# Moving the rounded activations of an fp32 matmul chain by 64 bytes within 256, with every other tensor kept at its byte

## Chip, cores and metric

One core of one Trainium2 chip runs the whole program in one launch. The metric is device time in microseconds (us), median over runs, and lower is better. Before the change it is 638.91 us, the median of 3 runs that lie between 638.78 and 639.15.

## What is computed

Three stages follow each other: windowed attention, a mixture of 4 experts with shares, and a block with a cosine. All data are fp32.

```python
# attention: 2 batches, 8 heads, 576 tokens, head size 64, each token sees itself and 63 before it
attn = softmax(where(mask, q @ k.T / 8, -1e9)); x = (attn @ v)        # as 1152 tokens x 512
p = domain_probs / (domain_probs.sum(-1) + 1e-9)                      # 1152 x 4
out = sum over e of p[:, e] * (relu(x @ w1[e]) @ w2[e])               # w1: 512 x 1024, w2: 1024 x 512
h = out @ w_in                                                        # w_in: 512 x 2048
result = (h * cos(h)) @ w_out                                         # w_out: 2048 x 512
```

## The kernel before

**Split products.** A weight or an activation `a` is held as two tensors of type float32r, a rounded part `a_hi` and what is left, `a_lo = a - a_hi`. A product `a b` is then three matmuls into one PSUM bank: `a_hi b_hi`, `a_hi b_lo` and `a_lo b_hi`. ScalarE writes the `_hi` tensors with a copy, VectorE or GpSimd writes the `_lo` tensors with a subtraction.

**The tensors.** `w_hi` and `w_lo` hold the 8 chunks (of 128 hidden units) of one block of weights, in 1024 columns each: 512 for the way up and 512 for the way down. `x_hi` and `x_lo` hold the tokens: 4 slices of 128 channels, 1152 tokens each. `hp_hi` and `hp_lo` hold the hidden values of four chunks for 384 tokens. For three of the experts, pairs of chunks are multiplied by a scheme with 7 products for 8 (`pair_product`). It needs sums of token blocks, `t_hi` and `t_lo`, and sums of weight blocks, `ex_hi` and `ex_lo`.

**The matmuls.** All of them have a stationary operand of 128 columns, which a weight load brings into the array, and a moving operand which is streamed through it.

- Up (`up_cells`, line 1270): stationary is a 128-column piece of `w`, moving are 384 tokens of `x`. A hidden chunk takes 12 matmuls (4 slices by 3).
- Up in pairs (`pair_product`, line 1314): stationary is a piece of `w` or `ex`, moving are 384 tokens of `x` or `t`. A product takes 6 matmuls.
- Down (`down_cells`, line 1297, and `pair_outputs`, line 1328): here the roles are the other way round. Stationary are 128 tokens of `hp`, moving are the 512 down columns of `w`. A hidden chunk takes 9 matmuls.

In a matmul the trace names the moving operand first: `bank<-x_hi,w_hi` is moving `x_hi` by stationary `w_hi`. Once the attention is done, TensorE goes to and fro between two chunks up (24 matmuls) and two chunks down (18), the down ones LAG = 3 chunks behind, so that ScalarE and VectorE have time to turn a bank into `hp_hi` and `hp_lo`. The order is written out by hand. Each engine has its own list of instructions, and semaphores join them.

**Where tensors lie.** SBUF tensors follow each other in the order in which they are declared, each start rounded up to 32 bytes. The first one, `w_hi`, starts at byte 16512 of each partition, that is at byte 128 modulo 256. `w_hi`, `w_lo`, `w_raw`, `x_hi` and `x_lo` are whole multiples of 256 bytes long, and so are all pieces into which matmuls cut them (512-byte pieces of `w` and `hp`, 1536-byte pieces of `x` and `t`). So each operand starts at the byte of its tensor, modulo 256.

Of the kernel before, what the change touches and what calls it, by code (L numbers as in the profile page):

```python
# [27 lines left out]
P = 128  # L28
# [12 lines left out]
E = 4  # L41
# [7 lines left out]
TILES = N // P  # L49
# [60 lines left out]
def build(nc, q, k, v, probs, weights, out):  # L110
    with ExitStack() as ctx:
        def sb(name, shape, dt=F32):
            return ctx.enter_context(nc.sbuf_tensor(name, shape, dt))
# [4 lines left out]
        w_hi = sb("w_hi", [P, FC, 2 * DM], F32R)  # L118
        w_lo = sb("w_lo", [P, FC, 2 * DM], F32R)
        w_raw = sb("w_raw", [P, STAGE, 2 * DM])  # L120
        x_hi = sb("x_hi", [P, DC, N], F32R)
        x_lo = sb("x_lo", [P, DC, N], F32R)
        p_tok = sb("p_tok", [P, E, TILES])
        half_pi = sb("half_pi", [P, 1])
        hp_hi = sb("hp_hi", [P, HP, TOK], F32R)
        hp_lo = sb("hp_lo", [P, HP, TOK], F32R)
        h_raw = sb("h_raw", [P, HP, TOK])
        p_now = sb("p_now", [P, NTOK, OC])
        ident = sb("ident", [P, P])
        mask = sb("mask", [P, 3, P])  # L130
        zeros = sb("zeros", [P, P])
# [25 lines left out]
        with ExitStack() as sums:  # L157
            def sum_sb(name, *shape):
                t = sums.enter_context(nc.sbuf_tensor(name, [P, *shape], F32R))
                return t[(slice(None),) * (len(shape) + 1)]  # L160

            t_hi = sum_sb("t_hi", 3, 2, TOK)
            t_lo = sum_sb("t_lo", 3, 2, TOK)
            ex_hi = sum_sb("ex_hi", GROUPS, EX * P)
            ex_lo = sum_sb("ex_lo", GROUPS, EX * P)
        c_u, c_k, c_r1, c_r2, c_abs, c_cos = (
# [1423 lines left out]
```

## Time and profile before

| | |
|---|---|
| median of 3 runs | 638.91 us |
| the profiled execution | 638.61 us, of which the span of instructions is 636.6 us |
| TensorE matmuls | 99% of the span, 3658 instructions |
| TensorE weight loads | 88% |
| VectorE, ScalarE, GpSimd | 47%, 41%, 43% |
| DMA | 36.73 MB in its main queue, 18.1% of the 16 engines' time |

Matmuls are pipelined, so one's duration in the trace (some 335 or 390 ns) is longer than the time from its start to the start of the next. That time, called the step below, is what a matmul costs in a stream, and it is read from starts in the timeline, or from the length of a run of matmuls in the chain of waits divided by their number.

### The profile page before, as it was taken

What the parts mean: (1) busy time and instruction counts of PE and PEld (TensorE: products, weight loads), DVE (VectorE), ACT (ScalarE), POOL (GpSimd) and SP (SyncE); (2) the same over time, 40 slices, a digit from 0 to 9 for tenths busy, and PEclk for the clock granted to TensorE, in tenths of its full rate; (3) what the DMA queues carried; (4) which work ended last, traced back from release to release, by engine and by line L of the source; (5) the groups of instructions that cost most, each with busy time, mean ns of one, the idle gap of its engine ahead of it and who ended that gap; (6) DMA issues with size and microseconds to landing.
All of it is one profiled execution on the core that took longest, in us unless ns stands there. A gap on an engine that the chain in (4) does not pass through costs nothing.

```text
span 636.6 us, 10169 instructions
## 1 busy us (share of the span) xinstructions
PE 629.4 (99%) x3658; PEld 562.4 (88%) x3658; DVE 301.9 (47%) x726; ACT 261.0 (41%) x558; POOL 271.7 (43%) x405
## 2 busy tenths in 40 slices
PE   7999999999999999999999999999999999999997
PEld 6877899989899999999998888988999999999996
DVE  5654431215433314432414443426775666766564
ACT  6885312233321223321223321246655467544542
POOL 6892246697710396720396720287000069400000
PEclk9999999999999999999999999999999999999999
DMA  9975000021220021120022220133100012001011
GB/s 271 280 237 187 8 1 0 1 66 67 68 66 1 1 66 66 66 66 0 1 67 66 67 66 1 32 101 100 34 0 1 2 39 94 1 0 49 0 51 50
DMA packets 23432, 37.25 MB, mean 59 GB/s; under 512 B 2784, under 2 KB 16096, under 8 KB 23392
## 3 DMA queue, kind: packets, MB, share of 16 engines
q1 hardware_dynamic: 23392, 36.73, 18.1%
q8 instruction: 24, 0.39, 0.3%
q14 instruction: 16, 0.13, 0.1%
HBM read 34.36 MB, written 2.36 MB: 58 GB/s over the span
## 4 chain that ended last, share of the span: by engine, by line
PE 97%; DVE 1%; DMA 1%; issue 0%; SPq 0%; POOL 0%; ACT 0%; DVEq 0%
PE bank L1270 31%; PE bank L1297 31%; PE bank L1328 16%; PE bank L1314 14%; PE bank L1248 2%; PE bank L1212 1%; PE bank L1237 1%; PE bank L1411 1%; DMA k_t<-in_k 1%; DVE s_sb L878 0%; DVE acc L1058 0%; DVE prob_t L927 0%; PE bank L1221 0%; SPq L322 0%; POOL prob L481 0%
## 5 line engine op out<-in xcount | busy, mean ns | idle before, releaser
L456 POOL TENSOR_TENSOR w_lo<-w_raw,w_hi 128x128 fp32r<-128x128 f32 (+1 forms) x244 | 144.9, 630 | 213.9 <-ACT w_hi L658 212.4
L1270 PE MATMUL bank<-x_hi,w_hi 128*128 128x384 f32 (+1 forms) x384 | 131.3, 342 | 0.0
L1270 PE MATMUL bank<-x_hi,w_lo 128*128 128x384 f32 (+1 forms) x384 | 129.2, 336 | 0.0
L1270 PE MATMUL bank<-x_lo,w_hi 128*128 128x384 f32 (+1 forms) x384 | 128.8, 335 | 0.0
L1297 PE MATMUL bank<-w_hi,hp_hi 128*128 128x512 f32 x288 | 114.8, 399 | 0.1
L1297 PE MATMUL bank<-w_hi,hp_lo 128*128 128x512 f32 x288 | 113.5, 394 | 0.0
L1297 PE MATMUL bank<-w_lo,hp_hi 128*128 128x512 f32 x288 | 112.2, 390 | 0.0
L1011 DVE TENSOR_TENSOR h_raw<-bank,h_raw 128x384 f32<-128x384 f32 x84 | 46.7, 556 | 91.8 <-PE bank L1314 91.7
L1270 PEld LDWEIGHTS bank<-x_hi,w_hi 128*128 128x128 f32 x384 | 72.2, 188 | 2.9 <-issue 0.5
L1270 PEld LDWEIGHTS bank<-x_lo,w_hi 128*128 128x128 f32 x384 | 72.2, 188 | 1.6
L942 DVE SCALAR_TENSOR_TENSOR hp_lo<-bank,hp_hi 128x384 fp32r<-128x384 f32 x48 | 26.5, 556 | 98.5 <-ACT hp_hi L690 57.5
L1270 PEld LDWEIGHTS bank<-x_hi,w_lo 128*128 128x128 f32 x384 | 72.1, 188 | 0.0
L1297 PEld LDWEIGHTS bank<-w_lo,hp_hi 128*128 128x128 f32 x288 | 54.1, 188 | 12.1
L682 ACT ACTIVATE hp_hi<-h_raw 128x384 fp32r<-128x384 f32 x48 | 25.2, 525 | 94.9 <-DVE h_raw L1011 94.9
L1297 PEld LDWEIGHTS bank<-w_hi,hp_hi 128*128 128x128 f32 x288 | 54.1, 188 | 10.8 <-issue 0.4
L1297 PEld LDWEIGHTS bank<-w_hi,hp_lo 128*128 128x128 f32 x288 | 54.3, 189 | 8.5
L1328 PE MATMUL bank<-w_hi,hp_lo 128*128 128x512 f32 x144 | 56.6, 393 | 0.0
L1328 PE MATMUL bank<-w_hi,hp_hi 128*128 128x512 f32 x144 | 56.6, 393 | 0.0
L1328 PE MATMUL bank<-w_lo,hp_hi 128*128 128x512 f32 x144 | 56.2, 390 | 0.0
L658 ACT ACTIVATE w_hi<-w_raw 128x1024 fp32r<-128x1024 f32 x40 | 42.0, 1051 | 11.7 <-PE bank L1297 11.7
L1077 DVE TENSOR_TENSOR h_raw<-c_cos,bank 128x384 f32<-128x384 f32 x48 | 26.6, 554 | 37.0 <-ACT c_cos L753 37.0
L751 ACT ACTIVATE c_abs<-c_r 128x384 f32<-128x384 f32 x48 | 25.2, 525 | 42.6 <-DVE c_r L1069 42.5
(112 smaller groups left out, 970.9 us busy)
## 6 DMA issues: line engine op xcount, KB each, us to landing
w_raw<-in_weights SPq DMA_DIRECT2D x43, 512.0 KB, 3.6
q_t<-in_q SPq DMA_DIRECT2D x12, 192.0 KB, 5.3
result<-acc SPq DMA_DIRECT2D x9, 256.0 KB, 2.1
w_raw<-in_weights SPq DMA_DIRECT2D x8, 256.0 KB, 6.0
k_t<-in_k SPq DMA_DIRECT2D x8, 224.0 KB, 5.6
v_w<-in_v SPq DMA_DIRECT2D x4, 384.0 KB, 4.8
v_w<-in_v SPq DMA_DIRECT2D x4, 320.0 KB, 6.2
k_t<-in_k SPq DMA_DIRECT2D x4, 192.0 KB, 4.4
```

The costliest lines, as they stand in the source:

```text
L456: last = nc.gpsimd.tensor_tensor(w_lo[:, f, at:at + part], raw[:, at - begin:at - begin + part], w_hi[:, f, at:at + part], ALU.subtract)
L658: nc.scalar.activation(w_hi[:, f, :], w_raw[:, f % STAGE, :], ACT.Copy).then_inc(w_hi_done, 1)
L682: nc.scalar.activation(hp_hi[:, i, :], h_raw[:, i, :], ACT.Relu).then_inc(pair_hi_done, 1)
L751: nc.scalar.activation(c_abs, c_r2, ACT.Abs).then_inc(cos_abs, 1)
L942: nc.vector.scalar_tensor_tensor(out=hp_lo[:, f % HP, :], in0=ps[:, 0:TOK], scalar=0.0, in1=hp_hi[:, f % HP, :], op0=ALU.max, op1=ALU.subt ...
L1011: nc.vector.tensor_tensor(h_raw[:, place, :], ps, h_raw[:, other, :], ALU.add).then_inc(pair_taken, 1)
L1077: nc.vector.tensor_tensor(h_raw[:, f % HP, :], c_cos, bank_h, ALU.mult).then_inc(cos_taken, 1)
L1248: last = nc.tensor.matmul(out_cell, v_w[:, r, WINDOW_OF[t][block_of], heads], prob_t[:, h, block_of // 2, at:at + WIN], start=True, stop=True)
L1270: last = nc.tensor.matmul(ps[:, 0:TOK], w[:, f, chunk(c)], x[:, c, token_cols(t)], start=c == 0 and i == 0, stop=c == DC - 1 and i == 2)
L1297: last = nc.tensor.matmul(y_ps[c][:, :], h[:, f % HP, chunk(c)], w[:, f, DM:2 * DM], start=f == 0 and i == 0, stop=f == FC - 1 and i == 2)
L1314: last = nc.tensor.matmul(bank[(g * PRODUCTS + j) % 2][:, 0:TOK], a, b, start=c == 0 and i == 0, stop=c == 1 and i == 2)
L1328: last = nc.tensor.matmul(pair_y[t][c][:, :], h[:, i, chunk(c)], w[:, f, DM:2 * DM], start=f == 0 and k == 0, stop=f == FC - 1 and k == 2)
```

## The change

Empty tensors are declared between others, and two small arrays (`p_tok`, the shares, and `half_pi`, a constant) go from between the tokens and the hidden values to behind `p_now`. No instruction is added, removed or moved on any engine, and shapes, semaphores and DMAs are the same. Only addresses differ.

```diff
         w_raw = sb("w_raw", [P, STAGE, 2 * DM])
+
+        sb("before_x", [P, 16])
         x_hi = sb("x_hi", [P, DC, N], F32R)
         x_lo = sb("x_lo", [P, DC, N], F32R)
-        p_tok = sb("p_tok", [P, E, TILES])
-        half_pi = sb("half_pi", [P, 1])
+        sb("before_hp", [P, 32])
         hp_hi = sb("hp_hi", [P, HP, TOK], F32R)
         hp_lo = sb("hp_lo", [P, HP, TOK], F32R)
         h_raw = sb("h_raw", [P, HP, TOK])
         p_now = sb("p_now", [P, NTOK, OC])
+        p_tok = sb("p_tok", [P, E, TILES])
+        half_pi = sb("half_pi", [P, 1])
+        sb("before_ident", [P, 16])
         ident = sb("ident", [P, P])
@@
+            sum_sb("before_t", 16)
             t_hi = sum_sb("t_hi", 3, 2, TOK)
             t_lo = sum_sb("t_lo", 3, 2, TOK)
+            sum_sb("before_ex", 48)
             ex_hi = sum_sb("ex_hi", GROUPS, EX * P)
             ex_lo = sum_sb("ex_lo", GROUPS, EX * P)
```

The starts that follow, in bytes of a partition modulo 256 (modulo 512 in brackets):

| tensors | before | after |
|---|---|---|
| `w_hi`, `w_lo`, `w_raw` | 128 (128) | 128 (128) |
| `x_hi`, `x_lo` | 128 (128) | 192 (192) |
| `t_hi`, `t_lo` | 128 (384) | 192 (192) |
| `ex_hi`, `ex_lo` | 128 (384) | 128 (384) |
| `hp_hi`, `hp_lo`, `h_raw`, `p_now` | 64 (320) | 64 (320) |
| `ident`, `mask`, `zeros`, `acc`, `q_t`, `k_t`, `v_w`, `s_sb`, `prob`, `prob_t`, `c_u` to `c_cos` | 128 (384) | 128 (128) |
| `p_tok` | 128 (128) | 128 (384) |

Moving less stationary, modulo 256, is therefore 0 before and 64 after in the up matmuls and in the pair products, and 64 both before and after in the down matmuls (`w` at 128 by `hp` at 64).

## Rows read from the trace of the kernel before

**Rows 1.** The page: span, TensorE's busy time, and its granted clock in 40 slices
```profile
span 636.6 us, 10169 instructions
...
PE 629.4 (99%) x3658; PEld 562.4 (88%) x3658; DVE 301.9 (47%) x726; ACT 261.0 (41%) x558; POOL 271.7 (43%) x405
...
PEclk9999999999999999999999999999999999999999
```
**Rows 2.** The page's chain that ended last, by engine and line
```profile
PE 97%; DVE 1%; DMA 1%; issue 0%; SPq 0%; POOL 0%; ACT 0%; DVEq 0%
PE bank L1270 31%; PE bank L1297 31%; PE bank L1328 16%; PE bank L1314 14%; PE bank L1248 2%; PE bank L1212 1%; PE bank L1237 1%; PE bank L1411 1%; DMA k_t<-in_k 1%; DVE s_sb L878 0%; DVE acc L1058 0%; DVE prob_t L927 0%; PE bank L1221 0%; SPq L322 0%; POOL prob L481 0%
```
**Rows 3.** Waits of TensorE: us in total, times, longest us
```profile
PE bank L1453 <- DVE zeros L858: 1.2, 1, 1.2
PE bank L1221 <- POOL prob L481: 0.7, 1, 0.7
PE bank L1212 <- DMA k_t<-in_k: 0.7, 1, 0.7
...
```
**Rows 4.** Groups of TensorE's instructions: count, busy us and mean ns, idle us
```profile
L1270 PE MATMUL bank<-x_hi,w_hi 128*128 128x384 f32 (+1 forms) x384 | 131.3, 342 | 0.0
...
L1297 PE MATMUL bank<-w_hi,hp_hi 128*128 128x512 f32 x288 | 114.8, 399 | 0.1
...
L1314 PE MATMUL bank<-x_hi,ex_hi 128*128 128x384 f32 x48 | 16.2, 337 | 0.0
L1314 PE MATMUL bank<-x_hi,w_hi 128*128 128x384 f32 x48 | 16.2, 337 | 0.0
...
L1314 PE MATMUL bank<-t_hi,w_hi 128*128 128x384 f32 x24 | 8.3, 345 | 0.0
```
**Rows 5.** The chain in order of time: start us, length us, line, matmuls in it
```profile
264.84 4.21 PE bank L1314 x24
...
391.80 4.17 PE bank L1270 x24
...
502.65 4.12 PE bank L1297 x18
506.77 4.19 PE bank L1270 x24
510.96 4.12 PE bank L1297 x18
```
**Rows 6.** Timeline of TensorE, one run up and one down: start us, length us
```profile
506.61 0.33 PE L1270 MATMUL bank<-x_hi,w_hi 128*128 128x384 f32 x1
506.78 0.34 PE L1270 MATMUL bank<-x_lo,w_hi 128*128 128x384 f32 x1
...
507.68 0.33 PE L1270 MATMUL bank<-x_hi,w_hi 128*128 128x384 f32 x1
...
510.80 0.39 PE L1297 MATMUL bank<-w_hi,hp_hi 128*128 128x512 f32 x1
...
514.92 0.33 PE L1270 MATMUL bank<-x_hi,w_hi 128*128 128x384 f32 x1
```
**Rows 7.** Timeline of the weight loads beside the first two of them
```profile
506.62 0.19 PEld L1270 LDWEIGHTS bank<-x_lo,w_hi 128*128 128x128 f32 x1
506.79 0.19 PEld L1270 LDWEIGHTS bank<-x_hi,w_lo 128*128 128x128 f32 x1
```
**Rows 8.** Groups of other engines that read or write the moved tensors
```profile
L530 POOL TENSOR_TENSOR h_raw<-h_raw,x_lo 128x768 f32<-128x768 f32 x6 | 11.1, 1857 | 0.5
L954 DVE TENSOR_TENSOR x_lo<-bank,x_hi 128x512 fp32r<-128x512 f32 x9 | 6.2, 690 | 12.3 <-ACT x_hi L737 12.3
L638 ACT ACTIVATE x_hi<-bank 128x384 fp32r<-128x384 f32 x11 | 5.4, 492 | 4.8 <-PE bank L1248 4.8
...
```
**Rows 9.** Waits of all engines, three of the longest: us in total, times, longest us
```profile
DVE h_raw L1011 <- PE bank L1314: 91.7, 56, 5.2
ACT hp_hi L690 <- PE bank L1270: 58.7, 24, 5.7
...
ACT c_u L744 <- PE bank L1270: 34.9, 22, 1.8
```

## The prediction

> **What bounds the kernel now.** I looked first at the page's head and at the granted clock. TensorE is busy for 99% of the span, and its clock is at the upper of its two levels, 2.4 GHz, in every slice, so no clock is left to win [rows 1]. Then I read the chain that ended last: 97% of it is TensorE, and the two kinds of matmul that the change touches, lines 1270 and 1314, make up 31% and 14%. The down matmuls of lines 1297 and 1328, whose operands keep their bytes, make up 31% and 16% [rows 2]. TensorE's own waits come third: the three longest are 1.2, 0.7 and 0.7 us, all in the first stage [rows 3]. So the time is the number of matmuls times the step of each, and a change that touches no instruction can act only through the step.
>
> The step is therefore what to measure. A run of 24 up matmuls takes 4.19 us in the chain of waits, 174.6 ns each, and a run of 18 down matmuls takes 4.12 us, 228.9 ns each [rows 5]. At 2.4 GHz and one column a cycle, 384 columns need 160.0 ns and 512 columns 213.3 ns. What is above that I call the stall: 14.6 ns up (9.1% of the streaming time) and 15.6 ns down (7.3%). TensorE did not wait for a semaphore in these runs. What does run beside each matmul is the weight load for the next one: it starts 0.01 us after the matmul and is 0.19 us long [rows 6, 7]. Both read SBUF. That they get in each other's way is a supposition, but it is the one by which an address could matter at all.
>
> The timeline of one up run shows more. Its first six matmuls go from 506.61 to 507.68, 178.3 ns each; the other eighteen go from 507.68 to 510.80, 173.3 ns each. The down run behind it, from 510.80 to 514.92, keeps to 228.9 ns [rows 6]. The operands of the second chunk up differ from those of the first only in which piece of `w` is stationary, so the same kind of matmul has two speeds, and the up stream, with moving and stationary at the same byte, needs six matmuls to fall into its better one. Of the 52 up runs of 24 in the chain, 39 take 4.19 us, the others 4.17, 4.18 or 4.21 [rows 5]. The down stream, whose moving operand lies 64 bytes further than the stationary one, shows no such start.
>
> **The change, part by part.**
>
> *Matmuls whose offset changes.* Line 1270 has three groups of 384; line 1314 has nine groups of 48 and three of 24 [rows 4]. That makes 1152 + 432 + 72 = 1656 matmuls, all of 384 columns. One nanosecond of step is 1.66 us, 0.26% of the time. The trace has no up matmul at offset 64, so its step is the unknown cost, and the rows bound it.
>
> - Lower bound: no stall at all, 160.0 ns. That is -14.6 ns x 1656 = -24.2 us.
> - Upper bound: the speed of the six unsettled matmuls, 178.3 ns, for all of them: +3.7 ns x 1656 = +6.1 us.
> - Nearest row: the down matmuls, which have this very offset with the same float32r type and the same 128-column weight load. They give two readings. If the stall is a share of the streaming time, it is 7.3% of 160.0 = 11.7 ns, a step of 171.7 ns. If it is a fixed time for each matmul, it is 15.6 ns, a step of 175.6 ns.
>
> I take the share. Two things speak for it: the down stream is steady from its first matmul on, so its offset is one at which the two readers keep out of each other's way from the start; and a share above 9% at offset 0 against 7.3% at offset 64 is the plainer reading of two streams that differ in length as well. Against it: a weight load has 128 columns in both, and if the stall arises only while it reads, it should not grow with the columns. That is why the other reading keeps a good chance. The term is (171.7 - 174.6) = -2.9 ns x 1656 = **-4.8 us**.
>
> *Pieces that move by 256 bytes.* `ex` lies 256 bytes off `w` modulo 512, and yet a matmul of `x_hi` by `ex_hi` has a mean of 337 ns, as one of `x_hi` by `w_hi` at the same line [rows 4]. So what moves by a multiple of 256 (`ident`, `acc`, `prob`, `q_t` and the rest) is costed at nothing. The down matmuls keep their bytes: nothing. At the seams, the last down matmul of a run stands beside a load of `w` or `ex` as before, and the last up matmul, one in 24, beside a load of `hp` at offset 128 in place of 64: one step in 24, too little for a term.
>
> *Other engines.* ScalarE writes `x_hi`, VectorE reads it and writes `x_lo`, and GpSimd reads both for the sums; these instructions take 492, 690 and 1857 ns and are few (11, 9 and 6 in the largest groups) [rows 8]. If an address made each of them 5% slower, that would be 5% of 11.1 + 6.2 + 5.4 us, about 1 us of work on engines that are busy for under half of the span [rows 1], beside matmuls. I put it at nothing; without that cover it would be +1 us. The number of bytes moved by DMA is the same.
>
> *Do the others keep up?* ScalarE waits 58.7 us for the up matmuls of line 1270 at one line and 34.9 at another, VectorE 91.7 us for the pair products [rows 9]. They wait for TensorE and not the reverse, with margins of a microsecond and more, so a gain of 0.07 us in a run of 24 passes through whole.
>
> The sum for the profiled execution is 638.6 - 4.8 = 633.8 us. Its time is 0.3 us under the median of the runs, so for the median I predict **634.1 us**.
>
> **The rivals.**
>
> 1. *The settled speed, without the start (chance 0.13).* Offset 64 only takes away the six slow matmuls, and all run at 173.3 ns: -1.3 ns x 1656 = -2.1 us, 636.8. The steady down runs speak for the first half; nothing says why the speed should then be the old one.
> 2. *Nothing happens (0.18).* The bytes don't matter, and the stall comes from something else, such as handing over from one matmul to the next. Then it is 638.9, with 0.3 either way. For it: 256 bytes make no difference. Against it: two speeds for equal work, which a fixed hand-over doesn't give. The Trainium skill, SBUF — State Buffer, "Who interferes with whom", says this outright: TensorE has two independent read ports, one for the moving operand and one for weight loads, and it never waits on anyone; by that page no byte offset costs anything and the change is worth 0. The trace here agrees only in part, since a step of 174.6 ns is 14.6 above its streaming time with no semaphore waited for.
> 3. *The down stall as a fixed time (0.22), the case on the slower side.* Up matmuls take over the 15.6 ns of the down ones and run at 175.6 ns: +1.0 ns x 1656 = +1.7 us, 640.6. It decides once the up step exceeds 175.4 ns (0.2% of the time, 1.28 us, is 0.8 ns of step). For it: the weight load is equally long in both [rows 7]. Against it: the up stream spends 18 of its 24 matmuls at 173.3.
> 4. *A stream that never settles (0.07).* At the new offset the readers keep colliding as in the first six matmuls: +6.1 us, 645.0. The down rows speak against it.
> 5. *The stall is gone (0.04).* 160.0 ns a step would be -24.2 us, 614.7. The down stream, at this very offset, still stalls for 15.6 ns. The Trainium skill, TensorE: Matmul & The Clock Gate, "Back-to-back issue gap", gives a warm isolated gap of N/2.4 + 2.5 ns, 162.5 ns here; an estimate from that page is -12.1 ns x 1656 = -20.0 us. No row here shows a stream so tight.
>
> **How the numbers follow.** My forecast has 0.36. No change can be told from noise within about 0.2%, that is 637.6 to 640.2. Faster are the forecast, rivals 1 and 5, less a little because the gains of the first two may come out small: 0.50. Within 0.2% are rival 2 and the small outcomes on both sides: 0.26. Slower are rivals 3 and 4, less the part of rival 3 near its threshold: 0.24. The range leaves out rivals 4 and 5 (0.11) and the outer ends of the forecast. It reaches up to rival 3 and 0.9 above it, 641.5. Down, it allows the forecast's stall of 11.7 ns to come out at 8 ns, another 3.7 x 1656 = 6.1 us less: 628.0.
>
> **What would show it.** In the changed kernel's trace, a run of 24 up matmuls should take 4.12 us in place of 4.19, the first six no longer than the others, and a down run 4.12 us as now. TensorE's waits stay as short as they are and the clock stays full. A run of 4.16 would be rival 1, one of 4.19 with a slow start rival 2, one of 4.21 rival 3. The prediction is wrong if the stall belongs to the weight load alone, or if a down run changes too, since its operands haven't moved; then the bytes act in some way that I don't see, on the seams between the streams for instance.

## The result: 0.3% slower, and where the time went

The changed kernel takes 640.92 us, the median of 8 runs (640.68 to 641.8), against 639.13 us for the kernel before in the same comparison (638.78 to 639.6, 8 runs). The ratio is 1.003, with a 95% interval of 1.0021 to 1.0039. The prediction was 634.1 us and a range from 628.0 to 641.5. So the time is inside the range, near its upper end, and the sign is the wrong one.

The page of the changed kernel, span, TensorE's busy time and granted clock:

```profile
span 639.8 us, 10169 instructions
...
PE 632.4 (99%) x3658; PEld 561.8 (88%) x3658; DVE 303.8 (47%) x726; ACT 260.8 (41%) x558; POOL 272.5 (43%) x405
...
PEclk9999999999999999999999999999999999999999
```

Against [rows 1], nothing but TensorE's 3 us more stands out, and the clock is as full as before. TensorE's waits for a semaphore are as short as before, the longest 1.2 us. The chain that ended last, in order of time (start us, length us, line, matmuls; six lines of insertion make line 1270 line 1276, 1297 line 1303, 1314 line 1320 and 1328 line 1334):

```profile
82.71 4.16 PE bank L1276 x24
...
500.81 4.16 PE bank L1276 x24
504.96 4.20 PE bank L1303 x18
509.16 4.16 PE bank L1276 x24
513.32 4.20 PE bank L1303 x18
...
628.18 7.01 PE bank L1303 x30
```

The same view of the kernel before, at the two ends of its stream:

```profile
81.69 4.17 PE bank L1270 x24
...
625.17 6.88 PE bank L1297 x30
```

Set beside [rows 5], an up run has gone from 4.19 to 4.16 us, and a down run from 4.12 to 4.20. The down matmuls are those whose operands kept their bytes. In the chain 47 up runs of 24 now take 4.16 us and 5 take 4.17; 50 down runs of 18 take 4.20, 12 take 4.13 or 4.14, and one takes 4.37 (4.39 before). The timeline tells the rest:

```profile
509.00 0.34 PE L1276 MATMUL bank<-x_hi,w_hi 128*128 128x384 f32 x1
...
510.04 0.34 PE L1276 MATMUL bank<-x_hi,w_hi 128*128 128x384 f32 x1
...
513.16 0.40 PE L1303 MATMUL bank<-w_hi,hp_hi 128*128 128x512 f32 x1
...
517.35 0.34 PE L1276 MATMUL bank<-x_hi,w_hi 128*128 128x384 f32 x1
```

The first six up matmuls take 1.04 us, and so does each six of the eighteen behind them: 173.3 ns a step from the start, where [rows 6] had 178.3 for the first six. The eighteen down matmuls take 4.19 us, 232.8 ns each, in place of 228.9.

From the first up run of the stream to the start of the last 30 down matmuls it is 628.18 - 82.71 = 545.47 us, and before it was 625.17 - 81.69 = 543.48: +1.99 us, which covers the 1.79 us between the medians. The profiled execution is 3.2 us longer than the one before; it is the longest of the eight, and 1.0 of that lies ahead of 82.71 us, in the attention stage with its waits, which the medians don't show.

By kind, from the starts in the two traces and leaving out steps in which a wait falls (over 200 ns up, over 240 down): the 1618 up steps sum to 280.5 us in place of 282.6, and the 1260 down steps to 292.8 in place of 288.8. That is -2.1 and +4.1 us.

### The profile page after: what moved, and what is told of

It is laid out like the page before. It is cut to its first block, busy times and chain, and to the rows that moved or that the text cites. A ratio compares the mean times of both kernels' runs of the same rounds, so it can differ in the third digit from the quotient of the medians.

```text
span 639.8 us, 10169 instructions
## 1 busy us (share of the span) xinstructions
PE 632.4 (99%) x3658; PEld 561.8 (88%) x3658; DVE 303.8 (47%) x726; ACT 260.8 (41%) x558; POOL 272.5 (43%) x405
## 4 chain that ended last, share of the span: by engine, by line
PE 96%; DMA 1%; DVE 1%; SPq 0%; issue 0%; POOL 0%; ACT 0%; DVEq 0%
PE bank L1303 31%; PE bank L1276 31%; PE bank L1334 16%; PE bank L1320 14%; PE bank L1254 2%; PE bank L1243 1%; PE bank L1218 1%; DMA w_raw<-in_weights 1%; PE bank L1417 1%; DVE s_sb L884 0%; DVE acc L1064 0%; POOL w_lo L470 0%; SPq L330 0%; SPq L328 0%; DVE prob_t L933 0%
## 5 line engine op out<-in xcount | busy, mean ns | idle before, releaser
L1303 PE MATMUL bank<-w_lo,hp_hi 128*128 128x512 f32 x288 | 114.1, 396 | 0.0
L1334 PE MATMUL bank<-w_lo,hp_hi 128*128 128x512 f32 x144 | 56.6, 393 | 0.0
```

The costliest lines, as they stand in the source:

```text
L1303: last = nc.tensor.matmul(y_ps[c][:, :], h[:, f % HP, chunk(c)], w[:, f, DM:2 * DM], start=f == 0 and i == 0, stop=f == FC - 1 and i == 2)
L1334: last = nc.tensor.matmul(pair_y[t][c][:, :], h[:, i, chunk(c)], w[:, f, DM:2 * DM], start=f == 0 and k == 0, stop=f == FC - 1 and k == 2)
```

## The experiments

### Streams alone, four bytes by four bytes

In a program of its own, TensorE runs nothing but streams of matmuls. First come 32 streams from rest, then cells of up (24), down (18), up, down, with every byte of x and h. In names, a to d stand for bytes 0, 64, 128 and 192, and `w` is at 128.

```python
for m, s, n in rest_runs:
    stream(xs[m], hs[s], n, 24, 2 + k % 2).then_inc(run_done, 1)
    ...
for x, h in mixed_runs:
    up(xs[x], 0)
    down(hs[h], 0)
    up(xs[x], 2)
    down(hs[h], 2).then_inc(run_done, 1)
```

> A kernel of matmul streams alone, on data of no meaning (the attention, the experts and the result are left out). x_a to x_d and h_a to h_d start at byte 0, 64, 128, 192 modulo 256. First 32 streams of 24 matmuls, each begun from rest: four moving bytes by four stationary bytes, with 384 and with 512 columns. Then 16 rows of up (24 matmuls, 384 columns), down (18, 512 columns), up, down, with w at byte 128, x at four bytes and h at four bytes. Theory 1, the seam: what a down run costs depends on how it is entered from the up run, by the byte of x against that of h. Begun from rest, 512 columns at moving 128 by stationary 64 have one step; in the rows, down runs with h at 64 take 4.12 us when x is at 128 and 4.20 us when x is at 192. Theory 2: the down run depends on its own operands alone; then all down runs with h at 64 take the same, whatever x is. On the first streams: if only the difference of the two bytes counts, cells of one difference agree within 1 ns a step; 384 columns at difference 0 settle at 173.3 ns, and at 64 as well.

Timeline of TensorE; a line is one run, and a run's cost is the start of the next less its own:

```profile
356.04 4.35 PE L88 MATMUL bank<-x_c,w 128*128 128x384 f32 x24
360.22 4.28 PE L95 MATMUL bank<-w,h_b 128*128 128x512 f32 x18
...
420.46 4.36 PE L95 MATMUL bank<-w,h_b 128*128 128x512 f32 x18
424.65 4.32 PE L88 MATMUL bank<-x_d,w 128*128 128x384 f32 x24
428.81 4.36 PE L95 MATMUL bank<-w,h_b 128*128 128x512 f32 x18
...
437.62 4.25 PE L95 MATMUL bank<-w,h_c 128*128 128x512 f32 x18
441.71 4.32 PE L88 MATMUL bank<-x_d,w 128*128 128x384 f32 x24
445.88 4.25 PE L95 MATMUL bank<-w,h_c 128*128 128x512 f32 x18
```

With the same `w` and the same `h_b`, a down run takes 4.19 us behind `x_d` (424.65 - 420.46) and 4.12 behind `x_c` (by the starts in ns, 4121). So matmuls alone, without another engine at work beside them, show both sides of the result: longer down runs, and up runs that are shorter by 28 ns. Down and up run together, from the start of one down run to that of the next, in ns:

| x at | h at 0 | h at 64 | h at 128 | h at 192 |
|---|---|---|---|---|
| 0 | 8407 | 8359 | 8302 | 8419 |
| 64 | 8374 | 8322 | 8320 | 8347 |
| 128 | 8366 | 8307 (kernel before) | 8307 | 8380 |
| 192 | 8366 | 8354 (the change) | **8254** | 8360 |

The change goes from 8307 to 8354 in it. Each cell was run once. The streams from rest agree to within 1.3 ns a step where the difference of moving and stationary is the same, whatever the bytes themselves (the very first is left out, as the clock was not yet full in it); their settled steps with 512 columns are 226.7 ns at difference 0, 228.9 at 64, 232.5 to 233.3 at 128, and 233.3 at 192. Begun from rest, 128 by 64 runs at 228.9 ns.

### Only the old bytes put back

```diff
-        sb("before_x", [P, 16])
-        sb("before_hp", [P, 32])
+        sb("before_hp", [P, 48])
-            sum_sb("before_t", 16)
-            sum_sb("before_ex", 48)
```

> The changed kernel with x and t put back to byte 128 modulo 256, all else as in the change: the small arrays behind p_now, and ident and all behind it 256 bytes further than before the change. Theory 1, the seam: the time is that of the kernel before, 639.0 within 0.3, down runs of 18 at 4.12 us and up runs of 24 at 4.19. Rival: the shift by 256 bytes or the place of the small arrays slowed the down runs; then they take 4.20 us and the time is 641 or above.

It takes 639.11 us against 639.13, a ratio of 1.0002 (0.9993 to 1.0012). Down runs are at 4.12 us, 53 of 63 exactly so. The place of the small arrays and the shift of `ident` and all behind it by 256 bytes cost nothing. The time comes from the bytes of x and t. The engines that write and read these tensors don't pay either: in the changed kernel the three instructions of [rows 8] take 492, 691 and 1850 ns, against 492, 690 and 1857.

### Only the high parts, only the low parts

```diff
+        sb("before_x", [P, 16])
         x_hi = sb("x_hi", [P, DC, N], F32R)
+        sb("before_x_lo", [P, 48])
         x_lo = sb("x_lo", [P, DC, N], F32R)
```

and the like for `t_hi` and `t_lo`; the second kernel has a 16-column pad ahead of the `_lo` tensors alone.

> Only x_hi and t_hi at byte 192, x_lo and t_lo at 128. The last matmul of each up run streams x_hi. Theory 1 in its narrow form (the last up matmul beside the first load of hp sets the down run's state): down runs take 4.20 us as in the changed kernel, time above 640. Rival, the state is built up over many up matmuls: down runs between 4.12 and 4.20, or a pattern of their own.

> Only x_lo and t_lo at byte 192, x_hi and t_hi at 128. Theory 1 in its narrow form: the last up matmul streams x_hi at 128, so down runs take 4.12 us as before the change, and if the up runs lose their slow start too, the time is 638.9 - 1.5 = 637.4. Rival, the state is built up over many up matmuls: down runs above 4.12 us and the time 639 to 641.

High parts only: 639.95 us, ratio 1.0013 (1.0003 to 1.0022). Low parts only: 639.18 us, 1.0002 (0.9992 to 1.0011). The chain of the first:

```profile
495.39 4.20 PE bank L1303 x18
499.58 4.17 PE bank L1276 x24
503.76 4.12 PE bank L1303 x18
507.88 4.17 PE bank L1276 x24
512.05 4.20 PE bank L1303 x18
```

The narrow form of the theory falls. Each up run here ends on the same matmul, with `x_hi` at 192, and yet the down runs go by turns at 4.20 and 4.12 us (22 of 62 at 4.20): both costs in one kernel, from the same instructions with the same bytes modulo 256. The turns could be those of the two pairs of slots of `hp` that the down runs use, and of the chunks of `w`. An up run of 12 settles that:

```profile
119.63 4.20 PE bank L1303 x18
...
128.00 4.12 PE bank L1303 x18
132.12 2.08 PE bank L1276 x12
134.20 4.12 PE bank L1303 x18
138.32 4.17 PE bank L1320 x24
142.49 4.20 PE bank L1303 x18
```

By the program's order these four down runs read slots 0 and 1, 2 and 3, 0 and 1, 2 and 3. The slots go on in turn and the costs don't, so each pair of slots is seen at both costs. What is handed on is more than the byte of the last matmul, and it reaches from one down run through a whole up run to the next. With the low parts only, the gain that I expected in the up runs came in 17 of 51 runs of 24, and down runs took 4.12 to 4.14.

### How long the state lasts, a pause, and narrow stationary operands

```python
for x in (2, 3):
    up(xs[x], 0)
    pause(long_down(hs[1]))          # 120 down matmuls
for x in (2, 3):
    pause(up(xs[x], 0))
    pause(down(hs[1], 0))
```

> Matmul streams alone (attention, experts and result are left out), w at byte 128. First up (24) with x at 128, then 120 down matmuls with h at 64; the same with x at 192. Theory 1, a state that lasts: the first 120 have a mean step of 228.9 ns, the second 233.3 ns, to the last one, with the same down operands. Rival: the slow start wears off within some matmuls and both end at 228.9. Then up, a pause, down (18), for x at 128 and at 192: theory 1 says that the pause wipes the state out, and both down runs settle at 228.9; the rival, that x at 192 harms h at 64 in some lasting way, says 233.3 for the second. Then 24 matmuls with 384 and with 512 columns, moving byte 128, stationary byte 128 and 64, and a stationary operand of 128, 64 and 32 columns: if the stall comes from the reads of the weight load, then at 128, 64, 32 columns the step of 384-column matmuls is 173.3, about 167, about 163; if it is a fixed hand-over, it stays 173.3.

The chain in order of time (L86 is up, L116 is the long down run):

```profile
20.00 6.96 PE bank L86 x24
26.95 27.48 PE bank L116 x120
...
54.61 4.43 PE bank L86 x24
59.04 28.01 PE bank L116 x120
```

120 down matmuls take 27.48 us behind x at 128 and 28.01 behind x at 192. The first up run takes 6.96 us because the clock rose to full only at 25.5 us, near its end, so the two entries differ in more than the byte; in the streams above, where both had the full clock, down runs of 18 show the same two costs. The steps of the down matmuls are 229, 232, 226 ns in turn in the first, mean 228.9, and 233, 233, 234 in the second, mean 233.3, down to the last one. So the stream has two steady cycles with the same operands, and in 120 matmuls it does not leave the one in which it starts. With a wait between up and down, the second is gone: both down runs then settle into steps of 226, 229 and 232 ns.

The third part went against the supposition of the prediction. Timeline, by width of the stationary operand (128*128, 128*64, 128*32):

```profile
133.24 5.73 PE L101 MATMUL bank<-x_c,h_c 128*128 128x512 f32 x24 [0.19 <-DVE tick L67]
139.16 5.74 PE L101 MATMUL bank<-x_c,h_c 128*64 128x512 f32 x24 [0.19 <-DVE tick L67]
145.09 5.74 PE L101 MATMUL bank<-x_c,h_c 128*32 128x512 f32 x24 [0.19 <-DVE tick L67]
```

The loads themselves get shorter, 188, 134 and 108 ns, and the settled steps don't. Settled steps, in ns, from the last twelve of each:

| moving columns, difference | 128 | 64 | 32 columns loaded |
|---|---|---|---|
| 384, 0 | 173.3 | 173.3 | 173.3 |
| 384, 64 | 173.3 | 176.2 | 175.6 |
| 512, 0 | 226.7 | 230.0 | 231.7 |
| 512, 64 | 228.9 | 228.3 | 231.7 |

A shorter load brings no step down by more than 0.6 ns and raises five of the eight, by 2.3 to 5.0. The stall is not the time that the weight load's reads take away.

### A grid of 32 bytes

```diff
-LETTERS = "abcd"
+LETTERS = "abcdefgh"
-                sb(f"pad_x_{a}", [P, 16])
+                sb(f"pad_x_{a}", [P, 8])
```

> Matmul streams alone (attention, experts and result are left out): up (24), down (18), up, down, with w at byte 128 and x and h each at the eight multiples of 32 modulo 256. The cells that the first grid of streams had come out the same: down run plus up run 8.307 us at x 128, h 64; 8.354 at x 192, h 64; 8.254 at x 192, h 128. If the memory is cut into pieces of 64 bytes, the new cells add nothing below 8.25; if its grain is 32 bytes or less, one of them may fall below. Theory of one limit for both streams: nothing is under 24 x 173.3 + 18 x 226.7 ns = 8.24 us.

Against the first grid, the three cells named came out within 1 ns, and fourteen of the sixteen within 8. The other two did not repeat: x at 0 by h at 0 was 29 ns shorter (8378; it is the first cell here, and the clock was not yet full when its first up run began) and x at 64 by h at 128 was 24 ns longer (8344). So the bytes alone do not always settle the cost of a cell, and 29 ns in a cell would be 1.8 us in the kernel. The shortest of the 64 is x at 96 by h at 128, 8247 ns, then x at 192 by h at 128, 8253. The longest is 224 by 224, 8458. Six of the eight bytes of h cost more than the kernel before's for every x: with h at 0, 32, 96, 160, 192 or 224 no cell is under 8340, and the eleven cells under that have h at 64 or 128. Nothing in steps of 32 bytes comes under 8.24 us, which is 24 x 173.3 + 18 x 226.7 ns, the best settled steps seen.

### The grid carried over to the kernel

```diff
         sb("before_hp", [P, n])      # n = 32 in the change; 48 puts hp at byte 128
```

The four kernels differ only in the pads ahead of `x_hi`, `t_hi`, `hp_hi`, `ident` and `ex_hi`.

> The changed kernel with hp moved to byte 128: x and t at 192, w by hp at difference 0. The first grid of streams gives 4.09 us for 18 down and 4.16 for 24 up matmuls, against 4.12 and 4.19 before the change and 4.20 and 4.16 after it. Theory 1: 0.053 us less than before for each up and down pair, some 63 of them, 3.3 us: 635.8, faster than both kernels. Rival, the streams alone don't carry over to the kernel, where other engines read SBUF too: 638 or above.

> All of w, x, t and hp at byte 128 modulo 256. In the first grid of streams this cell has the same length of an up and a down run as the kernel before has, 4.12 + 4.19 us, since its down runs start slowly and then run at 226.7 ns. Theory 1: 639.1 within 0.5. Rival, only the difference between moving and stationary operand counts, 226.7 ns for every down matmul: 1296 x 2.2 ns = 2.9 us less, 636.2.

> x and t at byte 96, hp at 128: the shortest cell of the grid of streams, 8.247 us for 18 down and 24 up matmuls, against 8.253 with x at 192 and 8.306 before the change. Theory 1: 63 x 0.059 = 3.7 us less than before, 635.4, about the same as with x at 192 (635.55). Rival, a difference of 32 bytes brings another conflict with the 512-byte pieces of ex in the pairs, which the grid has not: above 637.

> x, t and hp at byte 224: the longest cell of the grid of streams, 8.458 us for 18 down and 24 up matmuls against 8.306 before the change. Theory 1: 0.152 us more for each of some 63 pairs, 9.6 us: 648.6. Rival, in the whole kernel the streams are restarted by waits so often that the cells even out: under 644.

| x and t, hp | cell less 8307 ns, times 63 | expected | measured | ratio to before |
|---|---|---|---|---|
| 192, 128 | -3.3 us | 635.8 | 635.55 | 0.9941 (0.9927 to 0.9954) |
| 128, 128 | 0 | 639.1 | 639.35 | 0.9998 (0.9989 to 1.0007) |
| 96, 128 | -3.8 us | 635.4 | 634.97 | 0.9936 (0.9923 to 0.995) |
| 224, 224 | +9.5 us | 648.6 | 647.85 | 1.0135 (1.0119 to 1.015) |

All four came within 0.8 us of a figure that was worked out from a stream of matmuls alone. The change itself fits less well: its cell is 47 ns longer, times 63 is +3.0 us, and the medians show +1.8. The next experiment shows where a part of that goes. The row with all at 128 has a lesson of its own. Its down matmuls have difference 0, which from rest settles at 226.7 ns, and the kernel gains nothing: behind x at 128 a down run starts with nine steps of 231 ns in the mean, only then runs at 226.7, and takes 4.12 us as before. The chain with x at 192 and hp at 128:

```profile
496.04 4.16 PE bank L1274 x24
500.20 4.09 PE bank L1301 x18
```

It keeps the up run of the change, 4.16, and has a down run shorter than either kernel's, 4.09. The kernels with hp at 128 and x at 192 or at 96 are the version that beats both: 0.6% under the kernel before, and by their medians 0.8 and 0.9% under the changed one. The two differ by 0.0005 in ratio, which is within their intervals.

### Only the sums of tokens

```diff
+            sum_sb("before_t", 16)
             t_hi = sum_sb("t_hi", 3, 2, TOK)
             t_lo = sum_sb("t_lo", 3, 2, TOK)
+            sum_sb("before_ex", 48)
```

with x at byte 128, as before the change.

> Only t_hi and t_lo at byte 192, x at 128, hp at 64. In the pairs of the experts, down runs follow by turns on a product of x (a run of 24) and on one of t (a run of 18). Theory 1, the state in which the down run is entered: the 12 down runs behind a product of t take 4.20 us, those behind a product of x 4.12, so 12 x 0.075 = 0.9 us more, less some 0.3 for quicker starts of products: 639.9. Rival, the down runs slow down with x or with addresses as a whole: all stay at 4.12, or all rise.

It takes 639.54 us against 639.1, ratio 1.0007 (0.9998 to 1.0016), which is too little to tell by the time alone. The chain tells it:

```profile
178.06 3.14 PE bank L1318 x18
181.20 4.20 PE bank L1332 x18
185.39 4.19 PE bank L1318 x24
189.58 4.12 PE bank L1332 x18
```

A down run at line 1332 takes 4.20 us when the run ahead of it is one of 18, which ends on a product of `t`, and 4.12 when it is one of 24, which ends on a product of `x`. All 12 of each kind do so. The line and the bytes modulo 256 are the same; the slots of `hp` are not, but in the kernel before the same two kinds take 4.12 to 4.14 us. So the down run's cost is set at the seam, inside one kernel.

It is not set by the byte of `t` alone, though. In the changed kernel `t` lies at 192 too, and the chain there has it the other way round:

```profile
243.67 3.12 PE bank L1320 x18
246.78 4.13 PE bank L1334 x18
250.92 4.16 PE bank L1320 x24
255.08 4.20 PE bank L1334 x18
```

Of the 12 down runs behind a run of 18 that ends on `t`, 11 take 4.13 or 4.14 us there, and of the 12 behind a run of 24 that ends on `x`, 11 take 4.20. With x at 128 a product of `t` at 192 is followed by the slow cycle, and with x at 192 by the quick one. As with the high parts alone, what came before the last product counts as well. These 11 runs, some 0.06 us under 4.20 each, are by estimate 0.7 of the 1.2 us by which the grid overstates the change.

### Streams by number of columns

```python
rest_runs = [(2, s, n) for s in (2, 1, 0, 3) for n in (64, 128, 192, 256, 320, 384, 448, 512)]
```

> Streams of 48 matmuls, each begun from rest, with a moving operand of 64 to 512 columns in steps of 64 at byte 128 and a stationary operand of 128 columns at byte 128, 64, 0 and 192 (attention, experts and result are left out). The reading that the prediction took, the stall as a share of the streaming time: the step above columns / 2.4 GHz grows with the columns, at a difference of 64 about 7.3% of it for every length from 256 up. Rival, a fixed time: the best step is 13.3 ns above the streaming time at every length, at difference 0 above all (173.3 and 226.7 ns are both 13.3 above), and what a byte difference adds to it depends on length without a rule, because it is a cycle that the stream falls into.

The page shows the clock going down three times:

```profile
PEclk9999999999996559999997569999996559999997
```

Each time it fell while streams of 64 columns ran (97.0 us is the first) and was back during those of 192, so only streams from 256 columns up had the full clock throughout, and the table begins there. Settled step less columns / 2.4 GHz, in ns, from the last 24 steps of each stream:

| difference | 256 | 320 | 384 | 448 | 512 columns |
|---|---|---|---|---|---|
| 0 | 13.3 | 13.3 | 13.3 | 16.0 | 13.3 |
| 64 | 11.1 | 13.3 | 13.3 | 13.3 | 15.5 |
| 128 | 12.2 | 13.3 | 15.6 | 17.7 | 20.0 |
| 192 | 11.1 | 13.3 | 16.7 | 15.6 | 20.0 |

Timeline of the streams of difference 0 with 256, 448 and 512 columns:

```profile
49.28 6.03 PE L81 MATMUL bank<-x_c,h_c 128*128 128x256 f32 x48 [0.19 <-DVE tick L69]
...
71.78 10.00 PE L81 MATMUL bank<-x_c,h_c 128*128 128x448 f32 x48 [0.19 <-DVE tick L69]
81.98 11.19 PE L81 MATMUL bank<-x_c,h_c 128*128 128x512 f32 x48 [0.19 <-DVE tick L69]
```

The share falls: at difference 64 it is 10.4% of the streaming time with 256 columns and 7.3% with 512. A fixed time of 13.3 ns, which is 32 cycles at 2.4 GHz, fits nine of the twenty cells, and what is added or lacking beside it follows no simple rule in the columns. The stream of 384 columns at difference 192 settled at 176.7 ns here and at 173.3 in the first grid, with the same bytes: again two cycles for one pair of operands.

## Why the prediction was wrong

That the time lies in the range is luck: the range reached up to rival 3, whose mechanism did not come. Of the two terms, one was forecast at -4.8 us and came at -2.1, the other at nothing and came at +4.1.

**What bounds the kernel: right.** TensorE is the chain, its clock is full, and the time is the number of matmuls times the step. The other engines kept up in the gain with hp at 128 and x at 192, too: 3.8 us less came through, against the 3.3 expected.

**The up term: right in sign, mis-sized.** "If the stall is a share of the streaming time, it is 7.3% of 160.0 = 11.7 ns, a step of 171.7 ns" was to give -4.8 us. The up runs take 4.16 us and not 4.12, 173.3 ns a step in the mean, and the term measured is -2.1 us. That is rival 1 to the tenth of a microsecond. The streams by columns show that the share was the wrong reading: at a difference of 64 the stall is 13.3 ns at 384 columns, where the share gives 11.7, and 11.1 at 256, where it gives 7.8. Nor is this difference the better one for the down matmuls, as the prediction took from their even start: from rest they settle at 228.9 ns, against 226.7 at difference 0.

**The down term: this is the step that failed.** The prediction said "The down matmuls keep their bytes: nothing", and of the seams "one step in 24, too little for a term". Measured, the down matmuls cost +4.1 us, and turned -2.1 into +2.0. A matmul stream has a state that it hands on. With the same operands it runs at 228.9 or at 233.3 ns a step, for 120 matmuls and more, by how it was entered, and the new bytes of x enter it the bad way in most of the runs. The prediction named this among its signs of being wrong ("on the seams between the streams for instance"), but priced it at nothing. The rows of the kernel before held the warning: the six slow up matmuls of [rows 6] had the same bytes as the eighteen good ones, so the step was seen to depend on what came before. I read that as a cost of offset 0 alone and did not ask what it meant for the down runs.

**The pieces that move by 256 bytes, and the other engines: right.** The kernel with the old bytes put back has a ratio of 1.0002, and the three instructions of [rows 8] take what they took before.

**The rivals.** The time, 640.92, is that of rival 3 (640.6), but not by its mechanism: it had the up matmuls take over the stall of the down ones, at 175.6 ns, and they went the other way. Rival 2 is at most part of the truth: some 13 ns are left at the best bytes from 320 columns up, which could be what it called a hand-over, but bytes alone move the whole kernel by 2% (634.97 to 647.85 us). The Trainium skill, SBUF — State Buffer, "Who interferes with whom", has TensorE wait on nobody and its two read ports independent; whatever the ports do, the measurement decides against reading it as leave to ignore addresses.

**What stays open.** Which piece of hardware holds the state was not found. It is in TensorE's own path, since streams with the other engines at rest show it, and a wait wipes it out. It is not the length of the weight load's reads. No rule was found that says from the bytes which cycle a stream enters: the last byte doesn't, and two cells of the grid did not repeat. Whether the conflict is between moving and stationary reads at all is argued from the table by differences and not shown: no stream was run without weight loads.

## What to carry to other kernels

Where TensorE is the bound and its matmuls stand back to back, the bytes of the operands modulo 256 are worth a trial, 2% from the best to the worst here, and they must be judged for the whole round of streams and not for one kind of matmul: a change that makes one kind steady can put the next into a slower cycle. A short program of the streams alone, over a grid of bytes, foretold the kernel's time within 0.8 us for four choices of bytes; for the change itself, whose result was known by then, it is 1.2 us too high, so a gain or loss of a microsecond still has to be measured in the kernel. When equal instructions show two speeds in a trace, treat the speed as a state and ask what sets it before any step is called unchanged.

## What the hardware showed beyond that

- Two steady cycles of one stream: steps of 226, 229, 232 ns in turn, or of 233.3, with moving byte 128, stationary byte 64 and 512 columns. The first is also what a start from rest ends in.
- A kernel in which down runs go by turns at 4.20 and 4.12 us, with x_hi and x_lo at different bytes.
- The same product of `t` at byte 192 is followed by down runs of 4.20 us with x at 128, and of 4.13 or 4.14 with x at 192.
- At 256 columns a difference of 64 bytes is better than 0, by 2.2 ns a step; at 512 it is worse by 2.2. So the best difference depends on the number of columns.
- A stationary operand of 32 columns in place of 128 saves nothing in a back-to-back stream of 384 or 512 columns, and with 512 columns at difference 0 it costs 5.0 ns a step.
